# Attention scores head by head on 64x64 quarters of the tensor engine, from plain queries, with shorter first transfers

## The chip, the cores and the metric

The kernel runs on one core of a Trainium2 chip. A core has a tensor engine (PE in the rows; PEld is its weight load), a vector engine (DVE), a scalar engine (ACT), GpSimd (POOL) and a sync engine (SP) that here only issues transfers. The tensor engine has two clock levels, 1.2 and 2.4 GHz; "granted clock 1.00" is the upper one. The metric is the device time of one execution in microseconds, as the median of several runs.

## What is computed

Three stages follow each other: banded attention, a mixture of eight experts with the two best per token, and a dense block. The change is in the first only. Cut to that stage, and to the shape of the others:

```python
batch, n_heads, seq, head_dim = (4, 8, 576, 64)      # q, k, v: float32

def _attn_ref(q, k, v):
    window = 64
    scores = np.matmul(q, k.transpose(0, 1, 3, 2)) / np.sqrt(D)
    rel = pos[:, None] - pos[None, :]
    scores = np.where((rel >= 0) & (rel < window), scores, -1000000000.0)
    attn = np.exp(scores - np.max(scores, axis=-1, keepdims=True))
    attn = attn / (np.sum(attn, axis=-1, keepdims=True) + 1e-09)
    return np.matmul(attn, v)
...
x = attn_out.transpose(0, 2, 1, 3).reshape(B * S, H * D)      # 2304 x 512
x = _moe_ref(x=x, ...)     # router, top 2 of 8 experts, relu(x @ w1) @ w2
return _moe2_ref(x=x, ...) # g(x @ w_in) @ w_out
```

## The kernel before

**Tiling.** The queries of a sequence are cut into 9 blocks of 64 (i), for 4 batch entries (b): 36 steps, s = 4 i + b. A query sees at most the 64 keys of its own block and the 64 before. A step handles all 8 heads, as 4 pairs j of two heads (hi = 0 and 1); head 0 of a pair lies in partitions 0 to 63 and head 1 in 64 to 127, both in what goes in (partition = head dimension) and in the scores (partition = query).

**A step on PE.** First one bf16 matmul writes the mask (identity times mask, 512 columns) into one of three PSUM banks. Then `scores` (L936) adds, for each pair j, one matmul: the weights are a 128x128 block of `q_bd`, block-diagonal with the two heads' queries and zeros elsewhere, and the moving operand is the 128 keys (previous and own block) of both heads from `k_ring`. DVE takes the maximum (L699) and the bias (L704), ACT the exponentials (L552). PE transposes the probabilities (L947), DVE copies them back (L710), `values` (L959) makes eight matmuls with 64-column weights, whose outputs go to partitions 0 to 63 and 64 to 127 of one bank in turn, DVE divides by the sum (L723, `x_blk`), PE transposes x (L969), and every second step it makes the router's logits (L978). The order on PE is written out by hand: scores of step s, transposed probabilities of s-2, values of s-3, transposed x of s-4, logits after even steps. Every float32 matmul against data appears as two records in the trace, transposes as one.

**The first row of steps.** Steps 0 to 3 have no previous block. The kernel still multiplies 128 keys, with the second 64 (block 1, loaded for it at once) masked away; `first_k` therefore loads the keys of blocks 0 and 1, `first_v` the first 128 rows of v, both from ACT's queue. SP loads q, one transfer for each head of a pair, into the diagonal blocks of `q_bd` in runs of 64 numbers, which leaves the zeros that DVE wrote once (L684, L685) in place. Steps 0 and 1 wait for slices of their own, steps 2 and 3 share the third (`row0_loaded`). Each later row waits for `q_loaded` and `k_loaded`. In step b = 1 of each row SP waits until a row of scores is done, and loads q two rows and k three rows ahead. `keep_busy` is a string of matmuls of ones into an unused bank; 12 of them run before step 0.

**Weights beside attention.** POOL fetches the first expert's weights in 1 MB chunks into `stage`, the first two after the third and the sixth group of scores. In 16 pieces ACT casts them (`cast_piece`, L544, in steps 4, 6, ...), and DVE computes the low parts (`low_piece`, L691, in steps 5, 7, ... 35). After the last pieces POOL fetches chunks of the second expert; it converts those itself after the routing (L384). After attention come a routing stage on DVE, and then the experts, in which PE is busy nearly throughout.

Of the kernel before, what the change touches and what calls it, by code (L numbers as in the profile page):

```python
# [27 lines left out]
P = 128  # L28
# [17 lines left out]
def build(nc, qT, kT, vW, noise, w_gate, w_noise, w1, w2, w_in, w_out, out):  # L46
    BLOCKS, _, B, JQ = qT.shape
    Q = 64
    J = JQ // Q
# [31 lines left out]
    with ExitStack() as ctx:  # L81
# [36 lines left out]
        with ExitStack() as s1:  # L118
            sb = sb_in(s1)
            q_bd = sb("q_bd", [P, 2, B, J, 2, Q])  # L120
# [91 lines left out]
        k_loaded = [sem(f"k_loaded{c}") for c in range(4)]  # L212
        v_loaded = [sem(f"v_loaded{b}") for b in range(B)]
# [37 lines left out]
        def _(sp):  # L251
            def load_q(r):
                for hi in range(2):
                    rows = slice(64 * hi, 64 * hi + 64)
                    sp.dma_start(q_bd[rows, r % 2, :, :, hi].rearrange("p b j q -> p (b j) q"),
                                 qT[r, rows].rearrange("p b (j q) -> p (b j) q", j=J)).then_inc(q_loaded[r % 2], 16)
# [29 lines left out]
            for at in (slice(0, 1), slice(1, 2), slice(2, 4)):  # L286
                for hi in range(2):
                    rows = slice(64 * hi, 64 * hi + 64)
                    sp.dma_start(q_bd[rows, 0, at, :, hi].rearrange("p b j q -> p (b j) q"),
                                 qT[0, rows, at].rearrange("p b (j q) -> p (b j) q", j=J)  # L290
                                 ).then_inc(row0_loaded[at.start], 16)
            load_q(1)
            load_k(2)
# [56 lines left out]
        def _(pool):  # L350
# [104 lines left out]
            fetch_first(0, [(scored, 3), (scored, 6)])  # L455
# [82 lines left out]
        def _(act):  # L538
# [7 lines left out]
            def step(s):  # L546
# [16 lines left out]
                if s >= 4 and s % 2 == 0 and s < 4 + 8 * PIECES:  # L563
                    cast_piece((s - 4) // 2)
# [3 lines left out]
            def first_k(at):  # L568
                act.dma_start(k_ring[:, 0:3:2, at], kT[0:2, :, at].rearrange("i p b c -> p i b c")
                              ).then_inc(row0_loaded[at.start], 16)  # L570

            def first_v(b):
                act.dma_start(v_ring[:, b], vW[b, 0:P]).then_inc(v_loaded[b], 16)
# [107 lines left out]
        def _(dve):  # L681

            for c in range(2):
                nc.vector.memset(q_bd[64:128, c, :, :, 0], 0.0).then_inc(zeroed, 1)  # L684
                nc.vector.memset(q_bd[0:64, c, :, :, 1], 0.0).then_inc(zeroed, 1)  # L685

# [9 lines left out]
            def step(s):  # L696
# [30 lines left out]
                if s >= 5 and s % 2 and s < 5 + 8 * PIECES:  # L727
                    low_piece((s - 5) // 2)
# [176 lines left out]
        def _(pe):  # L905
# [7 lines left out]
            keep_busy(banks[7], 12)  # L913
# [263 lines left out]
```

## Time and profile before

| | us |
|---|---|
| median of 3 runs | 1104.11 (1103.42 to 1107.55) |
| profiled execution | 1104.26 |
| its span in the trace | 1102.7 |
| PE busy | 1084.7 (98%) |
| DVE, ACT, POOL busy | 350.1, 345.3, 355.2 |
| first scores, step 4, last logits of attention | from 8.06, 19.58, 121.00 |

The profiled execution is the one whose rows are shown; the time outside its span is 1.6 us. Times in the rows are microseconds from the start of the span. Matmuls are pipelined, so a record's duration includes latency that overlaps its neighbours, and the distance from one group's start to the next is the better measure of what a group costs.

### The profile page before, as it was taken

Reading aid. Unit: us, or ns where it says so; the run is one execution under the profiler, and the core shown is the slowest. Engines: PE = TensorE matmul, PEld = TensorE weight load, DVE = VectorE, ACT = ScalarE, POOL = GpSimd, SP = SyncE. Lnnn points to the kernel's source line nnn. Section 1 sums busy time; section 2 is a strip of 40 time slices with the busy share of each in tenths; the row PEclk is TensorE's granted clock in tenths of the full one; section 3 lists DMA queues with packets and bytes.
Section 4 is the critical chain, followed back from the end, with each engine's and each line's share of the span. In section 5 each row is a group of like instructions: output and inputs, shape, how many; then the busy total and the mean of one; then the engine's idle time right before and its main releaser. Section 6 shows DMA issues by size and latency. Waiting matters only on the chain.

```text
span 1102.7 us, 19553 instructions
## 1 busy us (share of the span) xinstructions
PE 1084.7 (98%) x6669; PEld 934.2 (85%) x6670; DVE 350.1 (32%) x685; ACT 345.3 (31%) x794; POOL 355.2 (32%) x230
## 2 busy tenths in 40 slices
PE   8999899999999999999999999999999999999998
PEld 6999568888888888888888887989989999899897
DVE  5888731122112211221122112424224132241321
ACT  4766212222222222222222221524325244252341
POOL 3000068559644628081725405921010110101000
PEclk8999989999999999999999999999999999999999
DMA  9886445995532514243333402220110201101000
GB/s 234 229 222 167 139 141 192 349 318 191 178 127 76 171 38 152 76 133 114 114 114 98 149 20 88 95 58 16 43 48 9 57 18 39 52 5 57 10 10 20
DMA packets 67844, 120.41 MB, mean 109 GB/s; under 512 B 25632, under 2 KB 30880, under 8 KB 67296
## 3 DMA queue, kind: packets, MB, share of 16 engines
q0 software_dynamic: 16688, 62.66, 17.4%
q1 hardware_dynamic: 37920, 33.67, 10.7%
q10 hardware_dynamic: 13200, 23.60, 6.6%
q8 instruction: 23, 0.38, 0.1%
q14 instruction: 13, 0.11, 0.0%
HBM read 87.14 MB, written 32.77 MB: 109 GB/s over the span
## 4 chain that ended last, share of the span: by engine, by line
PE 91%; POOL 4%; issue 3%; DMA 1%; DVE 0%; SPq 0%; ACT 0%; ACTq 0%; POOLq 0%; DVEq 0%
PE bank L1067 7%; PE bank L1065 7%; PE bank L1066 7%; PE bank L1050 7%; PE bank L1052 7%; PE bank L1051 7%; PE bank L1128 6%; PE bank L1130 6%; PE bank L1129 6%; PE bank L1115 6%; PE bank L1114 6%; PE bank L1113 6%; PE bank L1073 3%; PE bank L936 3%; PE bank L959 2%
## 5 line engine op out<-in xcount | busy, mean ns | idle before, releaser
L386 POOL TENSOR_TENSOR Wl<-stage,Wh 128x2048 fp32r<-128x2048 f32 x36 | 165.8, 4606 | 3.0
L1113 PE MATMUL bank<-zT_h,Wh 128*128 128x256 f32 x576 | 163.0, 283 | 1.0 <-DVE zT_l L873 1.0
L1115 PE MATMUL bank<-zT_h,Wl 128*128 128x256 f32 x576 | 163.0, 283 | 0.0
L1114 PE MATMUL bank<-zT_l,Wh 128*128 128x256 f32 x576 | 163.0, 283 | 0.0
L839 DVE COPY y_out<-bank 128x512 f32<-128x512 f32 x43 | 29.7, 692 | 359.7 <-PE bank L1067 342.4
L1050 PE MATMUL bank<-Wh,xT_h 128*128 x344 | 138.4, 402 | 1.1 <-POOL Wl L386 1.1
L1052 PE MATMUL bank<-Wh,xT_l 128*128 x344 | 134.6, 391 | 0.0
L1065 PE MATMUL bank<-Wh,hT_h 128*128 x344 | 133.9, 389 | 0.4 <-DVE hT_l L843 0.4
L1067 PE MATMUL bank<-Wh,hT_l 128*128 x344 | 134.2, 390 | 0.0
L1051 PE MATMUL bank<-Wl,xT_h 128*128 x344 | 133.8, 389 | 0.0
L1066 PE MATMUL bank<-Wl,hT_h 128*128 x344 | 133.8, 389 | 0.0
L620 ACT ACTIVATE hT_h<-bank 128x512 fp32r<-128x512 f32 x86 | 46.9, 596 | 260.9 <-PE bank L1073 153.4
L887 DVE SCALAR_TENSOR_TENSOR bank<-bank,square 128x512 f32<-128x512 f32 x72 | 50.4, 700 | 219.7 <-ACT square L659 219.7
L384 POOL CAST Wh<-stage 128x2048 fp32r<-128x2048 f32 x36 | 68.4, 1900 | 154.9 <-PE bank L1067 154.7
L502 POOL DMA_INDIRECT y_a<-y_sorted,pair_slot x18 | 17.2, 957 | 303.1 <-PE bank L1100 254.2
L1128 PE MATMUL bank<-Wh,gT_h 128*128 128x512 f32 x288 | 113.0, 393 | 0.2 <-POOL Wl L386 0.2
L1129 PE MATMUL bank<-Wl,gT_h 128*128 128x512 f32 x288 | 112.2, 390 | 0.0
L1130 PE MATMUL bank<-Wh,gT_l 128*128 128x512 f32 x288 | 112.2, 389 | 0.0
L1113 PEld LDWEIGHTS bank<-zT_h,Wh 128*128 128x128 f32 x576 | 110.5, 192 | 1.8 <-issue 1.5
L1114 PEld LDWEIGHTS bank<-zT_l,Wh 128*128 128x128 f32 x576 | 110.6, 192 | 0.3
L1115 PEld LDWEIGHTS bank<-zT_h,Wl 128*128 128x128 f32 x576 | 110.6, 192 | 0.0
L613 ACT ACTIVATE hid<-bank 128x512 f32<-128x512 f32 x86 | 51.4, 599 | 141.2 <-PE bank L1052 141.2
(154 smaller groups left out, 1674.0 us busy)
## 6 DMA issues: line engine op xcount, KB each, us to landing
stage<-w POOLq DMA_DIRECT2D x32, 1024.0 KB
y_sorted<-y_out ACTq DMA_DIRECT2D x43, 256.0 KB
x_in<-x_sorted ACTq DMA_DIRECT2D x39, 256.0 KB
x_sorted<-gath_b SPq DMA_DIRECT2D x20, 256.0 KB
x_sorted<-gath_a SPq DMA_DIRECT2D x19, 256.0 KB
x_rows<-x_blk SPq DMA_DIRECT2D x36, 128.0 KB, 3.0
out<-o_out SPq DMA_DIRECT2D x36, 128.0 KB, 2.2
q_bd<-qT SPq DMA_DIRECT2D x16, 256.0 KB, 4.3
```

Of the source, the lines that this page charges most:

```text
L1050: nc.tensor.matmul(H_ps[a][:], xT_h[:, u, k], high, start=(k == 0), stop=False)
L1051: nc.tensor.matmul(H_ps[a][:], xT_h[:, u, k], low, start=False, stop=False)
L1052: mm = nc.tensor.matmul(H_ps[a][:], xT_l[:, u, k], high, start=False, stop=(k == KD - 1))
L1065: nc.tensor.matmul(Y_ps[:], hT_h[:, k], high, start=(k == 0), stop=False)
L1066: nc.tensor.matmul(Y_ps[:], hT_h[:, k], low, start=False, stop=False)
L1067: mm = nc.tensor.matmul(Y_ps[:], hT_l[:, k], high, start=False, stop=(k == KF - 1))
L1113: nc.tensor.matmul(here, high, zT_h[:, k], start=(k == 0), stop=False)
L1114: nc.tensor.matmul(here, high, zT_l[:, k], start=False, stop=False)
L1115: mm = nc.tensor.matmul(here, low, zT_h[:, k], start=False, stop=(k == KD - 1))
L1128: nc.tensor.matmul(O_ps[u][:], gT_h[:, k, rows], Wh[:, 1, cols], start=(k == 0), stop=False)
L1129: nc.tensor.matmul(O_ps[u][:], gT_h[:, k, rows], Wl[:, 1, cols], start=False, stop=False)
L1130: mm = nc.tensor.matmul(O_ps[u][:], gT_l[:, k, rows], Wh[:, 1, cols], start=False, stop=(k == FC - 1))
```

## The change

The block-diagonal `q_bd` becomes `q_ring`, half as large, loaded by one transfer per slice with 256 to 1024 numbers in a row per partition. `scores` makes two matmuls for each pair of heads, each with a head's 64 partitions of q as 64x64 weights and the same 64 partitions of keys, into the 64 output partitions of that head. In steps 0 to 3 it multiplies 64 keys, and `values` contracts over 64 rows. The first k and v transfers shrink accordingly; k(1), q(1) and the second halves of v for the first row come from SP behind them. The zeroing memsets go. The warm-up matmuls are 9 instead of 12, and two more stand behind each of the first three groups of scores. POOL fetches its first two chunks after score groups 4 and 7, and the pieces of weights are cast and split two steps later.

```diff
-            q_bd = sb("q_bd", [P, 2, B, J, 2, Q])
+            q_ring = sb("q_ring", [P, 2, B, JQ])
...
             def load_q(r):
-                for hi in range(2):
-                    rows = slice(64 * hi, 64 * hi + 64)
-                    sp.dma_start(q_bd[rows, r % 2, :, :, hi].rearrange("p b j q -> p (b j) q"),
-                                 qT[r, rows].rearrange("p b (j q) -> p (b j) q", j=J)).then_inc(q_loaded[r % 2], 16)
+                sp.dma_start(q_ring[:, r % 2], qT[r]).then_inc(q_loaded[r % 2], 16)
...
+                sp.dma_start(q_ring[:, 0, at], qT[0, :, at]).then_inc(row0_loaded[at.start], 16)
+            load_k(1)
             load_q(1)
+            for b in range(B):
+                load_v(b, 1)
             load_k(2)
...
-            fetch_first(0, [(scored, 3), (scored, 6)])
+            fetch_first(0, [(scored, 4), (scored, 7)])
...
-                if s >= 4 and s % 2 == 0 and s < 4 + 8 * PIECES:
-                    cast_piece((s - 4) // 2)
+                if s >= 6 and s % 2 == 0 and s < 6 + 8 * PIECES:
+                    cast_piece((s - 6) // 2)
...
-                act.dma_start(k_ring[:, 0:3:2, at], kT[0:2, :, at].rearrange("i p b c -> p i b c")
-                              ).then_inc(row0_loaded[at.start], 16)
+                act.dma_start(k_ring[:, 0, at], kT[0, :, at]).then_inc(row0_loaded[at.start], 16)
...
-                act.dma_start(v_ring[:, b], vW[b, 0:P]).then_inc(v_loaded[b], 16)
+                act.dma_start(v_ring[0:Q, b], vW[b, 0:Q]).then_inc(v0_loaded[b], 16)
...
-            for c in range(2):
-                nc.vector.memset(q_bd[64:128, c, :, :, 0], 0.0).then_inc(zeroed, 1)
-                nc.vector.memset(q_bd[0:64, c, :, :, 1], 0.0).then_inc(zeroed, 1)
...
-                if s >= 5 and s % 2 and s < 5 + 8 * PIECES:
-                    low_piece((s - 5) // 2)
+                if s >= 7 and s % 2 and s < 7 + 8 * PIECES:
+                    low_piece((s - 7) // 2)
...
-            keep_busy(banks[7], 12)
+            keep_busy(banks[7], 9)
...
                 for j in range(J):
-                    mm = nc.tensor.matmul(
-                        S_ps[s % CH][:, P * j:P * j + P], q_bd[:, i % 2, b, j].rearrange("p a q -> p (a q)"),
-                        k_ring[:, even:odd + 1:odd - even, b, Q * j:Q * j + Q], start=False, stop=True,
-                        skip_group_check=True)
+                    for hi in range(2):
+                        rows, head = slice(Q * hi, Q * hi + Q), slice(Q * j, Q * j + Q)
+                        keys = k_ring[rows, 0, b, head] if i == 0 else k_ring[rows, even:odd + 1:odd - even, b, head]
+                        mm = nc.tensor.matmul(S_ps[s % CH][rows, P * j:P * j + (Q if i == 0 else P)],
+                                              q_ring[rows, i % 2, b, head], keys, start=False, stop=True,
+                                              skip_group_check=True)
...
+                rows = slice(0, Q if i == 0 else P)
...
-                        mm = nc.tensor.matmul(X_ps[s % 2][Q * hi:Q * hi + Q, Q * j:Q * j + Q], probsT[:, head],
-                                              v_ring[:, b, head], start=True, stop=True)
+                        mm = nc.tensor.matmul(X_ps[s % 2][Q * hi:Q * hi + Q, Q * j:Q * j + Q], probsT[rows, head],
+                                              v_ring[rows, b, head], start=True, stop=True)
...
                 if s < G:
                     scores(s)
+                if s < 3:
+                    keep_busy(banks[7], 2)
```

**Where instructions stand, before and after.** The first place is PE's queue at the start, up to the scores of step 3. Before:

```order
L909 MATMUL bank<-ones_b 128x512 x12
L932 MATMUL bank<-mask_first,ident_b 128x512
L936 MATMUL bank<-k_ring,q_bd 128x128 x4
L932 MATMUL bank<-mask_first,ident_b 128x512
L936 MATMUL bank<-k_ring,q_bd 128x128 x4
L932 MATMUL bank<-mask_first,ident_b 128x512
L936 MATMUL bank<-k_ring,q_bd 128x128 x4
L947 MATMUL bank<-ident,probs 128x128 x4
```

PE's queue at the same place after the change:

```order
L901 MATMUL bank<-ones_b 128x512 x9
L921 MATMUL bank<-mask_first,ident_b 128x512
L928 MATMUL bank<-k_ring,q_ring 64x64 x8
L901 MATMUL bank<-ones_b 128x512 x2
L921 MATMUL bank<-mask_first,ident_b 128x512
L928 MATMUL bank<-k_ring,q_ring 64x64 x8
L901 MATMUL bank<-ones_b 128x512 x2
L921 MATMUL bank<-mask_first,ident_b 128x512
L928 MATMUL bank<-k_ring,q_ring 64x64 x8
L901 MATMUL bank<-ones_b 128x512 x2
L938 MATMUL bank<-ident,probs 128x128 x4
```

Three of the ones matmuls left the front, six stand between the score groups, and each score group is eight matmuls of a quarter. The second place is one steady step on PE (scores, transposed probabilities, values, transposed x, logits). Before:

```order
L932 MATMUL bank<-mask_odd,ident_b 128x512
L936 MATMUL bank<-k_ring,q_bd 128x128 x4
L947 MATMUL bank<-ident,probs 128x128 x4
L959 MATMUL bank<-v_ring,probsT 64x64 x8
L969 MATMUL bank<-ident,x_blk 128x2x64 x2
L978 MATMUL bank<-w_gn,xT_blk 128x16 x4
```

The same steady step on PE after the change:

```order
L921 MATMUL bank<-mask_odd,ident_b 128x512
L928 MATMUL bank<-k_ring,q_ring 64x128 x8
L938 MATMUL bank<-ident,probs 128x128 x4
L954 MATMUL bank<-v_ring,probsT 64x64 x8
L964 MATMUL bank<-ident,x_blk 128x2x64 x2
L973 MATMUL bank<-w_gn,xT_blk 128x16 x4
```

The order within a step is the same; only the score group has other shapes, still with 128 keys each. The third place is DVE's queue at the end of attention, steps 37 and 38 of its loop. Before:

```order
L710 COPY probsT<-bank 128x512
L715 TENSOR_SCALAR rowsum_g<-rowsum 128x4
L718 RECIPROCAL rowinv<-rowsum_g 128x4
L723 TENSOR_TENSOR x_blk<-bank,rowinv 128x256
L715 TENSOR_SCALAR rowsum_g<-rowsum 128x4
L718 RECIPROCAL rowinv<-rowsum_g 128x4
L723 TENSOR_TENSOR x_blk<-bank,rowinv 128x256
```

DVE's queue at the same place after the change:

```order
L702 COPY probsT<-bank 128x512
L707 TENSOR_SCALAR rowsum_g<-rowsum 128x4
L710 RECIPROCAL rowinv<-rowsum_g 128x4
L715 TENSOR_TENSOR x_blk<-bank,rowinv 128x256
L683 TENSOR_TENSOR Wl<-stage,Wh 128x512
L707 TENSOR_SCALAR rowsum_g<-rowsum 128x4
L710 RECIPROCAL rowinv<-rowsum_g 128x4
L715 TENSOR_TENSOR x_blk<-bank,rowinv 128x256
```

The last low piece of weights (`Wl`) now stands between the last two blocks of x.

## Rows read from the trace of the kernel before

**Rows 1.** The page's first part: busy us, share of the span, instructions.

```profile
PE 1084.7 (98%) x6669; PEld 934.2 (85%) x6670; DVE 350.1 (32%) x685; ACT 345.3 (31%) x794; POOL 355.2 (32%) x230
```

**Rows 2.** Busy time by stretch, two steady steps, and the first of them alone.

```profile
core 0: us, PE busy (x) PEld busy (x) DVE busy (x) ACT busy (x) POOL busy (x), PEclk, DMA share, GB/s
59.82:62.35 2.53, 2.53 (x34) 2.26 (x31) 2.46 (x6) 1.70 (x9) 0.00 (x0) 1.00 0.82 279
...
59.82:65.68 5.86, 5.86 (x72) 5.32 (x70) 4.88 (x14) 4.01 (x20) 0.00 (x0) 1.00 0.51 160
```

**Rows 3.** Waits from 30 to 100 us: who waited for whom, total, times, longest.

```profile
PEld bank L959 <- issue: 4.0, 24, 0.2
```

**Rows 4.** PE in order of time, a steady step: start, duration of the group, instruction.

```profile
59.82 0.38 PE L932 MATMUL bank<-mask_even,ident_b 128*128 128x512 bf16 x1
60.04 1.05 PE L936 MATMUL bank<-k_ring,q_bd 128*128 128x128 f32 x8
60.93 0.60 PE L947 MATMUL bank<-ident,probs 128*128 128x128 f32 x4
61.46 0.69 PE L959 MATMUL bank<-v_ring,probsT 128*64 128x64 f32 x16
62.07 0.44 PE L969 MATMUL bank<-ident,x_blk 128*128 128x128 f32 x2
62.35 0.96 PE L978 MATMUL bank<-w_gn,xT_blk 128*128 128x16 f32 x8
```

**Rows 5.** PE in order of time, from the start to step 4.

```profile
1.23 4.17 PE L909 MATMUL bank<-ones_b 128*128 128x512 bf16 x12 [1.23 <-POOL ones_b L410]
8.06 0.59 PE L932 MATMUL bank<-mask_first,ident_b 128*128 128x512 bf16 x1 [2.66 <-POOL upper L434]
...
10.96 0.61 PE L932 MATMUL bank<-mask_first,ident_b 128*128 128x512 bf16 x1 [0.61 <-DMA q_bd<-qT]
...
13.94 0.61 PE L932 MATMUL bank<-mask_first,ident_b 128*128 128x512 bf16 x1 [0.67 <-DMA q_bd<-qT]
...
19.58 0.39 PE L932 MATMUL bank<-mask_odd,ident_b 128*128 128x512 bf16 x1
```

**Rows 6.** POOL, DVE and ACT in order of time, around step 0.

```profile
2.73 0.72 POOL L418 TENSOR_SCALAR_AFFINE_SELECT mask_first<-mask_first 64x128 bf16<-64x128 bf16 x2
...
10.39 0.69 DVE L699 TENSOR_REDUCE negmax<-bank 128x4 f32<-128x512 f32 x1 [4.68 <-PE bank L936]
...
12.61 0.21 ACT L552 ACTIVATION_READ_ACCUMULATOR probs<-bank,bias 128x1 f32 x1
```

**Rows 7.** DMA from 0 to 8 us: packets; issues, KB each, median us to landing.

```profile
DMA packets 1774, 1.44 MB, mean 180 GB/s; under 512 B 916, under 2 KB 1428, under 8 KB 1774
...
q_bd<-qT SPq DMA_DIRECT2D x4, 64.0 KB, 6.1
```

**Rows 8.** DVE and PE in order of time, the end of attention.

```profile
119.07 0.42 DVE L723 TENSOR_TENSOR x_blk<-bank,rowinv 128x256 f32<-128x256 f32 x1
...
119.89 0.42 PE L969 MATMUL bank<-ident,x_blk 128*128 128x128 f32 x2
```

**Rows 9.** Value and score records by line, 60 to 66 us: ns min/median/max.

```profile
L959 PE MATMUL bank<-v_ring,probsT x32: 222/222/270, 61.5 to 65.3; 128*64 128x64 f32 x32
...
L936 PE MATMUL bank<-k_ring,q_bd x17: 270/275/275, 60.0 to 65.9; 128*128 128x128 f32 x17
```

**Rows 10.** Busy time by stretch near the start; columns as in rows 2.

```profile
7.00:9.00 2.00, 0.94 (x4) 0.88 (x5) 0.00 (x0) 0.00 (x0) 1.59 (x7) 0.63 1.07 334
8.00:11.50 3.50, 2.83 (x11) 2.39 (x12) 0.86 (x2) 0.18 (x1) 2.20 (x9) 0.50 1.11 301
12.00:15.00 3.00, 2.33 (x11) 1.95 (x11) 0.86 (x2) 1.58 (x11) 0.00 (x0) 0.50 1.41 196
7.00:8.00 1.00, 0.00 (x0) 0.00 (x0) 0.00 (x0) 0.00 (x0) 0.80 (x4) 0.76 1.03 359
17.00:18.00 1.00, 1.00 (x7) 0.91 (x6) 0.82 (x2) 0.78 (x5) 0.86 (x1) 0.62 1.04 397
```

**Rows 11.** POOL in order of time: the second expert's first chunk.

```profile
154.94 1.90 POOL L384 CAST Wh<-stage 128x2048 fp32r<-128x2048 f32 x1
```

More of the change, by code:

```diff
@@ L212, in build @@
         k_loaded = [sem(f"k_loaded{c}") for c in range(4)]
+        v0_loaded = [sem(f"v0_loaded{b}") for b in range(B)]
         v_loaded = [sem(f"v_loaded{b}") for b in range(B)]
@@ L286, in _ @@
             for at in (slice(0, 1), slice(1, 2), slice(2, 4)):
[L287 to L290, printed above, removed]
-                                 ).then_inc(row0_loaded[at.start], 16)
+                sp.dma_start(q_ring[:, 0, at], qT[0, :, at]).then_inc(row0_loaded[at.start], 16)
+            load_k(1)
             load_q(1)
+            for b in range(B):
+                load_v(b, 1)
             load_k(2)
@@ L919, in scores @@
                 if i == 0:
-                    pe.wait_ge(row0_loaded[min(b, 2)], 48)
+                    pe.wait_ge(row0_loaded[min(b, 2)], 32)
                 elif b == 0:
-                    pe.wait_ge(q_loaded[i % 2], 32 * ((i + 1) // 2))
-                    if i >= 2:
-                        pe.wait_ge(k_loaded[i % 4], 16 * ((i + 2) // 4 if i % 4 >= 2 else i // 4))
-                if s in (0, B):
-                    pe.wait_ge(zeroed, 2 * i + 2)
+                    pe.wait_ge(q_loaded[i % 2], 16 * ((i + 1) // 2))
+                    pe.wait_ge(k_loaded[i % 4], 16 * (i // 4 + (1 if i % 4 else 0)))
                 if s in (B, 2 * B):
@@ L952, in values @@
                 pe.wait_ge(pT_copied, s + 1)
-                pe.wait_ge(v_loaded[b], 16 * max(i, 1))
+                if i == 0:
+                    pe.wait_ge(v0_loaded[b], 16)
+                else:
+                    pe.wait_ge(v_loaded[b], 16 * i)
+                rows = slice(0, Q if i == 0 else P)
                 if s >= 2:
@@ L998, in _ @@
             pe.wait_ge(const_ready, ALL_CONSTANTS)
-            pe.wait_ge(zeroed, 5)
+            pe.wait_ge(zeroed, 1)
             keep_busy(banks[4], 28)
```

1 line of the change is left out of this document (removed).

## The prediction

> **What bounds the kernel now.** I read the page first: the tensor engine (PE) is busy 98% of a span of 1102.7 us, so time is lost or won where PE's work gets longer or shorter, or where PE stands still [rows 1]. The change touches only the attention stage, the first 120 us. I read that stage in three pieces.
>
> The steady part is steps 4 to 35. In two consecutive steps, from 59.82 to 65.68 us, PE is busy 5.86 of 5.86 us at a granted clock of 1.00, DVE 4.88 and ACT 4.01 [rows 2]. The only waits on PE's side between 30 and 100 us are 0.2 us at a time of its weight loads in front of the value products, and they wait for no other engine [rows 3]. So PE's queue is the bound here: a step without logits takes 2.53 us, one with them 0.80 more (5.86 for the two), and every 0.1 us on PE in each of 32 steps is 3.2 us of the total.
>
> The start is bound by loads. PE idles 2.66 us before its first mask matmul at 8.06; the next two start at 10.96 and 13.94, and for these the trace names the q transfer as releaser [rows 5]. Step 4, the first on the steady rhythm, starts at 19.58. At the first mask the trace names a POOL instruction, but the constants that it needs (seven, ending with the two mask selects at 2.73) were ready by 3.5 us [rows 6]; what came last must be the transfers. The first four q transfers, of only 64 KB each, land a median of 6.1 us after issue [rows 7].
>
> The end of attention, to about 122 us, is a chain of latencies in which DVE and PE alternate [rows 8].
>
> **Part 1: scores on quarters, steps 4 to 35.** Before, four matmuls of 128x128 weights make 8 records; they hold PE from 60.04 to 60.93, 0.89 us, or 0.111 us a record [rows 4]. After, eight matmuls, each 64 rows by 64 columns of weights, still stream 128 keys, so they make 16 records as long as the old ones. The new q columns have no zeros, but the streaming is per key and not per useful product: if two quarters never ran at once the group would double. No row of this trace shows two quarters on different rows. The nearest are the value products: 128-row by 64-column halves, left and right in turn. A single record there takes 222 ns against 275 for a score record [rows 9], so 53 ns less for half of the streamed columns: 64 keys' worth of streaming is 53 ns, and 128 are 107. Sixteen value records alone would need 16 x 0.053 = 0.85 us; the group goes from 61.46 to the next group's start at 62.07, 0.61 us [rows 4]. So halves that write different partitions of one bank do overlap in pairs. I take it that the diagonal quarters do too: 16 x 0.107 / 2 = 0.85 us of streaming, what it was before.
>
> What comes on top is read from the same value group. The transposes before it are 4 records of 0.107 (0.43 us) and start at 60.93, so they should end at 61.36, and values start at 61.46: 0.10 us. From 61.36 to 62.07 is 0.71 us for 0.43 us of paired streaming (half of 0.85): 0.28 us over. The transposes of x behind it take 0.28 (62.07 to 62.35) where two records are 0.21, another 0.06 [rows 4]. Between groups of full-width weights there is next to nothing: mask to scores 0.22 for 512 bf16 columns (0.213), scores to transposes 0.89 for 0.85. So entering and leaving the split array costs 0.28 to 0.34 us per group. The scores group sits between a full-width mask and full-width transposes, so it pays the same: 0.85 + 0.28 to 0.34 = 1.13 to 1.19 us against 0.89, so +0.24 to +0.30, and I add about 0.01 because the half-filled first and last slot is longer for a longer record. I take **+0.28 us a step, x 32 = +9.0 us**. Bounds: no switching cost and full overlap, +0 to +0.03 a step (0 to +1 us); no overlap, 16 x 0.111 = 1.78 plus the 0.2 of the two switches, 1.98, so +1.09 a step (+35 us).
>
> Cover: DVE has 4.88 us of work in 5.86, ACT 4.01 [rows 2]. A longer PE step only widens that margin.
>
> **Part 2: the start.** Four edits act here. The first transfers carry half the keys and half the values of the first row of steps: q 0.5 MB, k 0.5, v 0.5 instead of 0.5, 1.0 and 1.0. The q transfer is one per slice instead of two, with runs of 1 KB or 4 KB per partition instead of 256 B. From 12 to 15 us, with the 256-byte runs of q(1) in flight, the DMA share was 1.41 at only 196 GB/s; from 7 to 9 us it was 1.07 at 334 [rows 10]. The four memsets of q's zeros leave DVE, which then waited 4.68 us for the first scores [rows 6]: worth nothing. The score products of steps 0 to 3 stream 64 keys: 8 x 2 records at 53 ns.
>
> Step 2 needs all of q(0) and k(0), 1.0 MB, and what the two queues interleave with it, some 0.4 MB of v and k(1). By rows 7, 1.44 MB had moved by 8.0 us, so step 2 can start near **7.5 us** instead of 13.94, steps 0 and 1 near 4.7 and 6 (twelve warm-up matmuls end at 5.4 in rows 5, the last ones at 0.22 each as the mask in rows 4, so nine end at about 4.7). Step 4 needs k(1) and q(1) too: 2.5 MB in all, which had moved at about 11.5 us before (1.44 MB to 8.0, then 3.5 us at 301 GB/s, 1.0 MB more [rows 10]), with under 1 us to land: **12.2 us** instead of 19.58. The engines' latency allows that: from the end of step 0's scores, where the first reduction starts, to its last exponential are 2.4 us (10.39 to 12.82) [rows 6], so the exponentials of step 0 end at about 8.2, transposes 0 and scores 3 follow from 8.6 to 9.8, and scores 4, after transposes 1 and values 0, could start at 11.2. The six extra warm-up matmuls (0.43 us a pair) fall in these waits. The gain is 19.58 - 12.2 = **-7.4 us**. Upper end -8.4, if only the latencies bind. Lower end -4: the granted clock was below full in the slice from 7 to 8 us, after PE had been idle from 5.4, and back in the slice from 17 to 18 [rows 5, 10]. A cold step costs some 2.5 us more; if the clock falls again in the short gaps between the first steps, one or two of the steps from 4 on run at half clock.
>
> SP's queue: k(1), q(1), four v transfers, k(2), k(3) and the small loads stand ahead of the first per-step wait. They are 14 issues where there were 13, of fewer descriptors; the first that has to wait is needed at step 8 only, near 23 us. POOL's first weight chunk waits for four score groups instead of three, but that falls at about 10 instead of behind the third group's end near 16, so it meets k(1), q(1) and v. ACT needs it in step 6 only, near 20 us. Nothing.
>
> **Part 3: the pieces of weights, two steps later.** The last DVE piece (0.68 us) moves from step 35 to step 37, between the x block of step 34 and that of step 35. There x_blk of step 35 runs from 119.07 to 119.49, and PE, busy with logits, takes it up at 119.89 [rows 8]. The piece puts x_blk's end at about 120.2, PE follows at 120.3: **+0.4 us** (0 to +0.7). POOL's next chunk is fetched some 3 us later and first converted at 154.9 [rows 11], so it is not late. From there on the program is the same, and the whole shift arrives at the end.
>
> **Sum.** -7.4 + 9.0 + 0.4 = +2.0 us on the profiled execution's 1104.26 (span 1102.7 and 1.6 around it), which is 0.15 above the median of 1104.11. **Forecast 1106.3.**
>
> **Rivals.** (a) *The quarters take turns.* The two quarters of a pair write one bank from different rows of the array; the value halves, the only rows that show an overlap, share both bank and rows [rows 4]. If quarters don't overlap, part 1's bound holds: +35 us for 32 steps, with -7.4 and +0.4: **1132**. Page "TensorEngine Tiling (Array Packing)" of the Trainium skill, Gotcha 1, is a rule for it: different row tiles cannot access the same PSUM bank simultaneously; no row here shows two row tiles. It decides once more than an eighth of the pairs fail to overlap (0.81 us x 32 = 26 us for all of them; 3.5 would carry the sum past +5.5). Against it: the two quarters write different partitions, as the halves of rows 4 do. 0.15.
> (b) *Switching is free here.* If the 0.28 to 0.34 us of the value group belongs to its three semaphore waits and not to the split, the scores, which wait for nothing after the mask, pay +1 us in all: -7.4 + 1 + 0.4 = **1098.3**. Against it: the 0.06 behind the group is no wait, and groups headed by a mask or transposes wait as well at almost no cost. 0.20.
> (c) *The start gives little*, as k(1) and q(1) land with the chunk in front of them or the clock falls: -4 + 9 + 0.4 and a little, **1110 to 1111**. 0.12.
> The forecast's own case has 0.53, from 1104 (+0.24 a step, -8.4) to 1110.5 (+0.34, a start of -5).
>
> **How the numbers follow.** A measurement of this kernel tells about 0.5% (5.5 us) from no change: 1098.6 to 1109.6. Rival (b) straddles the lower edge: 0.12 of it is faster, and 0.06 I take from the forecast's case for a gain that I don't see, with fewer q packets: faster 0.18. Slower is (a), most of (c), and the forecast's upper tail: 0.15 + 0.08 + 0.07 = 0.30. Same 0.52. The range of 8 in 10 leaves out (a) and the outer ends: 1098 to 1114. The likeliest case alone is 1104 to 1110.5.
>
> **What would show it.** In the new trace: score records in pairs, 16 in about 1.0 us, and transposes of the probabilities starting about 1.17 us after the first quarter; if they start 1.9 or more after, (a). A plain step of 2.81, one with logits of 3.62; if 2.55, (b). The mask of step 4 at 12.2; at 15 or later, (c). x_blk of step 35 behind a weight piece. I would be wrong beyond all this if PE waited for DVE in the steady part, or if the stages behind attention did not start with the same delay.

## The result

| | before | after |
|---|---|---|
| median of 5 runs, us | 1104.11 (1103.42 to 1108.55) | 1113.78 (1111.72 to 1114.69) |
| profiled execution, its span, us | 1104.26, 1102.7 | 1111.87, 1110.3 |
| mask of step 4 | 19.58 | 15.33 |
| steady: a plain step, and two steps with logits once | 2.53, 5.86 | 2.80, 6.42 |
| transposed x of step 35 | 119.89 | 124.52 |
| first routing matmul on PE | 128.79 | 135.94 |

The ratio over all the runs is 1.0068 (95% interval 1.005 to 1.0086), so the kernel is slower by some 7.5 us. The two medians lie further apart, 9.7 us, because the five runs of before fall in two clumps, three from 1103.42 to 1104.11 and two at 1107.55 and 1108.55 (the last section comes to that). The forecast was no change, at 1106.3. The median lies just inside the range of 1098 to 1114, and beyond the likeliest case's own 1110.5.

The page's first part (engine: busy us, share of the span, instructions), against [rows 1], has 8.7 us more of PE work, about what 32 steps got longer:

```profile
PE 1093.4 (98%) x6960; PEld 926.6 (83%) x6961; DVE 347.6 (31%) x681; ACT 345.0 (31%) x794; POOL 355.2 (32%) x230
```

Busy time by stretch, a plain step and then two steps, against [rows 2]:

```profile
core 0: us, PE busy (x) PEld busy (x) DVE busy (x) ACT busy (x) POOL busy (x), PEclk, DMA share, GB/s
59.49:62.29 2.80, 2.80 (x41) 2.09 (x39) 2.69 (x8) 1.57 (x9) 0.00 (x0) 1.00 0.48 162
59.49:65.91 6.42, 6.42 (x88) 5.06 (x86) 4.93 (x14) 4.01 (x20) 0.00 (x0) 1.00 0.42 121
```

PE in order of time in the same step (start, duration of the group, instruction), against [rows 4]:

```profile
59.49 0.38 PE L921 MATMUL bank<-mask_even,ident_b 128*128 128x512 bf16 x1
59.80 1.09 PE L928 MATMUL bank<-k_ring,q_ring 64*64 64x128 f32 x16
60.82 0.66 PE L938 MATMUL bank<-ident,probs 128*128 128x128 f32 x4
61.41 0.69 PE L954 MATMUL bank<-v_ring,probsT 128*64 128x64 f32 x16
62.02 0.44 PE L964 MATMUL bank<-ident,x_blk 128*128 128x128 f32 x2
62.30 0.96 PE L973 MATMUL bank<-w_gn,xT_blk 128*128 128x16 f32 x8
```

Start to start, against before: mask to scores 0.31 (was 0.22), scores to transposes 1.02 (0.89), transposes to values 0.59 (0.53). These three make the 0.28. PE is never idle, at a granted clock of 1.00.

PE at the start, against [rows 5]:

```profile
5.04 0.63 PE L921 MATMUL bank<-mask_first,ident_b 128*128 128x512 bf16 x1
...
7.05 0.38 PE L921 MATMUL bank<-mask_first,ident_b 128*128 128x512 bf16 x1
...
11.31 0.39 PE L921 MATMUL bank<-mask_first,ident_b 128*128 128x512 bf16 x1 [2.73 <-DMA k_ring<-kT]
...
15.33 0.39 PE L921 MATMUL bank<-mask_odd,ident_b 128*128 128x512 bf16 x1
```

Steps 0 and 1 start at 5.04 and 7.05, where 4.7 and 6 were forecast, and step 2 at 11.31 and not at 7.5. The DMA issues from 0 to 8 us (count, KB each, median us to landing), against [rows 7], name what it waited for:

```profile
q_ring<-qT SPq DMA_DIRECT2D x1, 256.0 KB, 4.8
k_ring<-kT ACTq DMA_DIRECT2D x1, 256.0 KB, 8.8
```

The third slice of q landed 4.8 us after its issue, the slice of k of the same size 8.8 us.

The end of attention, DVE and then PE in order of time, against [rows 8]:

```profile
122.69 0.42 DVE L715 TENSOR_TENSOR x_blk<-bank,rowinv 128x256 f32<-128x256 f32 x1
123.03 0.68 DVE L683 TENSOR_TENSOR Wl<-stage,Wh 128x512 fp32r<-128x512 f32 x1
...
124.04 0.42 DVE L715 TENSOR_TENSOR x_blk<-bank,rowinv 128x256 f32<-128x256 f32 x1
```

```profile
123.45 0.96 PE L973 MATMUL bank<-w_gn,xT_blk 128*128 128x16 f32 x8
124.52 0.44 PE L964 MATMUL bank<-ident,x_blk 128*128 128x128 f32 x2
125.65 1.64 PE L973 MATMUL bank<-w_gn,xT_blk 128*128 128x16 f32 x8 [0.69 <-ACT xT_blk L558]
127.12 8.98 PE L901 MATMUL bank<-ones_b 128*128 128x512 bf16 x28
135.94 0.23 PE L999 MATMUL bank<-picked,upper 128*128 128x152 bf16 x1
```

Behind x come the last logits, 28 filler matmuls of ones, and the routing's first matmul, which needs `picked` from DVE (133.66 to 133.97). In the trace of before the same rows, not shown so far, read:

```profile
119.08 0.96 PE L978 MATMUL bank<-w_gn,xT_blk 128*128 128x16 f32 x8
119.89 0.42 PE L969 MATMUL bank<-ident,x_blk 128*128 128x128 f32 x2
121.00 1.06 PE L978 MATMUL bank<-w_gn,xT_blk 128*128 128x16 f32 x8 [0.69 <-ACT xT_blk L561]
121.91 6.20 PE L909 MATMUL bank<-ones_b 128*128 128x512 bf16 x28
128.79 0.24 PE L1002 MATMUL bank<-picked,upper 128*128 128x152 bf16 x1 [0.68 <-DVE picked L770]
```

From x of step 35 to the routing it is 8.90 us there and 11.42 here. The stretches of after say why: the granted clock was at the lower level from about 126 us to 132.8, in before's trace at 1.00 until the routing.

```profile
126.00:128.00 2.00, 2.00 (x10) 1.45 (x10) 0.54 (x2) 0.00 (x0) 0.00 (x0) 0.50 0.71 283
```

The same 28 fillers took 8.98 us instead of 6.20, and now PE, not DVE, came last: DVE's `picked` ends 9.45 us behind x instead of 8.85, which is 0.6 of the 2.5 us, and PE's overrun is the rest. So the trace's account, after against before: -4.25 at step 4; +8.7 over the 31 steps to the mask of step 35 (114.50 against 110.06), which makes +4.44 there; +4.36 at the values of step 35 (122.42 against 118.06); +4.63 with the piece of weights; +7.15 at the routing; +7.6 at the end of the span.

### The profile page after: what moved, and what is told of

It reads as the page before. It is cut to its first block, busy times and chain, and to the rows that moved or that the text cites. A ratio compares the mean times of both kernels' runs of the same rounds, so it can differ in the third digit from the quotient of the medians.

```text
span 1110.3 us, 20125 instructions
## 1 busy us (share of the span) xinstructions
PE 1093.4 (98%) x6960; PEld 926.6 (83%) x6961; DVE 347.6 (31%) x681; ACT 345.0 (31%) x794; POOL 355.2 (32%) x230
## 4 chain that ended last, share of the span: by engine, by line
PE 93%; POOL 3%; DVE 1%; issue 1%; DMA 1%; ACT 0%; ACTq 0%; DVEq 0%; POOLq 0%
PE bank L1047 7%; PE bank L1049 7%; PE bank L1062 7%; PE bank L1064 7%; PE bank L1048 7%; PE bank L1063 7%; PE bank L1125 6%; PE bank L1127 6%; PE bank L1126 6%; PE bank L1112 6%; PE bank L1111 6%; PE bank L1110 6%; PE bank L1070 3%; PE bank L928 3%; PE bank L954 2%; PE bank L938 2%
```

## Experiments

The theory behind the first four runs: 0.28 us a step belongs to the score group's quarters alone and is the price of going from full-width weights to split ones and back. Rivals: the longer steps come from the loads or the moved pieces, or from the new record shape whatever its neighbours. Each group of runs had its own runs of before beside it: 19 with a median of 1106.06 for the first four, 25 with 1105.09 for the next four, 24 with 1105.91 for the last three. Ratios are comparable across groups, medians less so. "Better than the changed kernel" below is the difference of the two ratios, in us of 1104; the changed kernel's own interval is 1.005 to 1.0086, so a difference of less than some 3 us is not shown by the times alone.

**Quarters alone.** The kernel before with plain queries and the new score loop; transfers, sizes and everything else as before.

```diff
-            q_bd = sb("q_bd", [P, 2, B, J, 2, Q])
+            q_ring = sb("q_ring", [P, 2, B, JQ])
...
-                    mm = nc.tensor.matmul(
-                        S_ps[s % CH][:, P * j:P * j + P], q_bd[:, i % 2, b, j].rearrange("p a q -> p (a q)"),
...
+                    for hi in range(2):
...
+                        mm = nc.tensor.matmul(S_ps[s % CH][rows, P * j:P * j + P], q_ring[rows, i % 2, b, head],
...
```

> The kernel before with one part of the change alone: the scores as eight quarter products from plain q (q still loaded in runs of 256 bytes, all first transfers, warm-ups and weight pieces as before). Theory: the +0.28 us a step on PE is the score group alone (0.89 us to about 1.2), so steps 4 to 35 give +9.0 us, step 4 still starts near 19.6, and the time is 1104.1 + 9 = 1113, plus up to 2.5 if the clock falls behind attention as it did in the changed kernel. Rival: part of the +0.28 comes from elsewhere (the weight pieces two steps later, other DMA traffic); then the plain step stays under 2.75 us and the time under 1110.

Measured: 1114.41 us (1113.35 to 1115.74), ratio 1.0087 (1.0064 to 1.0111), which is +9.6 us. PE in its steady step:

```profile
59.69 0.38 PE L927 MATMUL bank<-mask_even,ident_b 128*128 128x512 bf16 x1
59.99 1.09 PE L933 MATMUL bank<-k_ring,q_ring 64*64 64x128 f32 x16
...
62.49 0.38 PE L927 MATMUL bank<-mask_even,ident_b 128*128 128x512 bf16 x1
```

2.80 from mask to mask, as in after. The quarters alone make the loss. Step 4 starts at 18.32 in this trace, 1.26 earlier than in before's, though nothing in its loads was changed: one profiled start is not yet its program's start.

**Start alone.** The changed kernel with the block-diagonal queries and full-width weights back.

```diff
-            q_ring = sb("q_ring", [P, 2, B, JQ])
+            q_bd = sb("q_bd", [P, 2, B, J, 2, Q])
...
+                    mm = nc.tensor.matmul(S_ps[s % CH][:, P * j:P * j + (Q if i == 0 else P)],
+                                          q_bd[:, i % 2, b, j].rearrange("p a q -> p (a q)"), keys, start=False,
...
```

> The changed kernel with the other part alone: block-diagonal q and four 128x128 score products a step as before (64 keys in steps 0 to 3), with the shortened first transfers, the fillers and the later weight pieces. Theory: steady steps are back at 2.53 and 3.33 us; step 4 starts 4 us earlier than before if what delayed it is the order and share of the transfers, so 1104.1 - 4 + 0.3 = 1100. Rival: the plain q transfers were what brought the 4 us (the q slices of 256-byte runs land late again), then step 4 starts at 17 or later and the time is 1102 to 1104.

Measured: 1104.80 us (1101.64 to 1106.42, 10 runs), ratio 0.9993 (0.9978 to 1.0009): the whole start is worth 0.8 us, between 2.4 of gain and 1 of loss. The time expected above is 4.8 lower, and the times include the later pieces (some +0.3). A plain step is back at 2.52 (60.26 to 62.78). At the start no load holds PE up for long, and step 4 comes before the rival's 17, but PE is slow:

```profile
5.96 1.80 PE L940 MATMUL bank<-k_ring,q_bd 128*128 128x64 f32 x8
...
14.70 1.00 PE L940 MATMUL bank<-k_ring,q_bd 128*128 128x64 f32 x8
...
16.69 0.39 PE L934 MATMUL bank<-mask_odd,ident_b 128*128 128x512 bf16 x1
```

The same eight records take 1.80 us in step 0, 1.81 in steps 1 and 2, and 1.00 in step 3. The masks of steps 1 and 2 take 0.63 us, as at the lower clock in before's trace (0.61 at a granted clock of 0.50), and this trace's first clock record, at the upper level, begins at 13.9 us, where after's begins at 6.5. So the lower clock lasted longer here than in after's trace, with the same nine warm-up matmuls; why is open. Step 4 starts at 16.69, 2.9 earlier than before and not 7.4. Quarters and start together, +9.6 - 0.8 = +8.8, agree with the +7.5 of the whole change within the intervals.

**By rows.** The changed kernel with the four upper quarters first and the four lower ones then.

```diff
-                for j in range(J):
-                    for hi in range(2):
+                for hi in range(2):
+                    for j in range(J):
```

> The changed kernel, with the eight quarter products of a step in another order: the four of the upper rows first, then the four of the lower rows. Theory: two quarters overlap only because neighbours in the queue lie on different quarters, starts being in order; four in a row on one quarter run one after the other, 16 x 0.107 = 1.7 us, +0.8 us a step, 1113.8 + 27 = 1140. Rival: the queue finds the other quarter's work by itself, then the time stays within 3 us of 1113.8.

Measured: 1125.78 us (two runs, 1123.78 and 1127.78), ratio 1.019 (1.0155 to 1.0226). Its score group:

```profile
61.31 1.58 PE L928 MATMUL bank<-k_ring,q_ring 64*64 64x128 f32 x16
62.82 0.66 PE L938 MATMUL bank<-ident,probs 128*128 128x128 f32 x4
```

1.51 us to the transposes against 1.02: neither theory's number, but in between. The starts of the single records show why. In after's trace they are two files of eight, both from 59.80 or 59.81 to 60.61 or 60.62. Here the upper quarters' file runs from 61.31 to 62.13 and the lower ones' from 61.81 to 62.62: the second starts 0.49 us late, which is the whole difference, and while three records of the first have yet to start. So the two files overlap in part even when they stand one behind the other in the queue, and wholly only when they alternate. Without any overlap the streaming alone would be 16 x 0.107 = 1.7 us, an estimate from [rows 9].

**Values first.** The changed kernel with the values of step s-3 ahead of the transposes of step s-2, so that the two split groups (scores and values) are neighbours.

```diff
-                if 2 <= s < G + 2:
-                    transposed_probs(s - 2)
                 if 3 <= s < G + 3:
                     values(s - 3)
+                if 2 <= s < G + 2:
+                    transposed_probs(s - 2)
```

> The changed kernel with the value products placed in front of the transposes of probabilities in each step on PE, so that the two split groups (64x64 scores, 128x64 values) stand next to each other: three changes of the array's division a step instead of four. Theory: the price is the change of division, so one of four falls away, -0.1 us a step or more, -3 to -5 us: 1109 to 1111. Rival 1: a change between two kinds of split costs the same as two changes from and to the full array, or the price lies in the split groups' own records: no difference. Rival 2: the later transposes make DVE's copy late, and PE waits: slower.

Measured: 1105.41 us (1102.81 to 1108.77, 10 runs), ratio 1.0003 (0.9988 to 1.0017), 7.2 us better than the changed kernel, where 3 to 5 were expected. PE in its steady step:

```profile
62.17 0.38 PE L921 MATMUL bank<-mask_even,ident_b 128*128 128x512 bf16 x1
62.48 1.09 PE L928 MATMUL bank<-k_ring,q_ring 64*64 64x128 f32 x16
63.50 0.69 PE L954 MATMUL bank<-v_ring,probsT 128*64 128x64 f32 x16
64.12 0.66 PE L938 MATMUL bank<-ident,probs 128*128 128x128 f32 x4
...
64.83 0.38 PE L921 MATMUL bank<-mask_odd,ident_b 128*128 128x512 bf16 x1
```

2.66 a step instead of 2.80, 4.5 us over 32 steps; from the mask of step 4 (17.10) to the transposed x of step 35 (120.99) it is 103.89 us against 109.19, so another 0.8 comes at the end, where the chain of latencies is shorter. The remaining 1.9 of the 7.2 is within the intervals.

**The same swap in the kernel before** (one run) is the control. There the scores are full width, and the swap joins nothing.

> The kernel before, with the value products in front of the transposes of probabilities on PE. Here the scores are full-width, so the array is divided and joined once a step in either order. Theory (the price is per change of division): a plain step stays within 0.05 us of 2.53. Rival (the order itself, or the waits at the head of the value products, made the 0.14 us a step that the same swap gave the changed kernel): 2.40 or less.

Measured: 1107.64 us in one run. A step with logits goes from 60.71 to 64.05, 3.34 us, and [rows 2] give 5.86 - 2.53 = 3.33: no change. From scores to values it is 0.99 us, where [rows 4] have 0.89 from scores to transposes: the 0.10 us ahead of the value group moved with it. So, as far as one trace of each kernel shows, the swap's 0.14 us is the price of one change from split weights to full ones and back, which is what the theory says. This trace shows another thing too: it has the fall of the clock behind attention, without any quarter.

```profile
121.49 1.89 PE L978 MATMUL bank<-w_gn,xT_blk 128*128 128x16 f32 x8 [0.69 <-ACT xT_blk L561]
123.22 8.49 PE L909 MATMUL bank<-ones_b 128*128 128x512 bf16 x28
```

**What held the third slice of k.** Two theories: SP's later transfers (k(1), q(1), v) compete with it for the DMA engines; or it stands in ACT's own queue behind the first slice of v. First run: SP holds its later loads until the slice has landed. Second: k's slice goes ahead of v in ACT's queue.

```diff
+            sp.wait_ge(row0_loaded[2], 32)
             load_k(1)
             load_q(1)
```

> The changed kernel, with SP's second group of transfers (k(1), q(1), the second halves of v, k(2), k(3) and the small loads) issued only when the third slices of q(0) and k(0) have landed. In the changed kernel step 2 starts at 11.31 us and waits for the third slice of k, which lands 8.8 us after its issue. Theory: that slice shares the DMA engines with what SP issues behind q(0); held back, it lands by about 8 and step 2 starts at 7.5 to 8.5, step 4 at 12 to 13.5, so about 2 to 3 us less than the changed kernel in the trace. Rival: the slice is held up in ACT's own queue behind the first slice of v, then step 2 still starts after 10, and step 4 gets later as k(1) and q(1) come late.

```diff
-                first_v(0)
                 first_k(slice(2, 4))
+                first_v(0)
```

> The changed kernel, with ACT issuing the third slice of k in front of the first slice of v instead of behind it; SP's transfers as in the changed kernel. Theory (SP's transfers take the share): step 2 still starts at 10 or later. Rival (ACT's own queue): step 2 starts by 9.

Measured: held loads 1112.29 us (1109.35 to 1115.69), ratio 1.0057 (1.0034 to 1.0079); k first 1109.06 us (1108.04 to 1113.10), ratio 1.0044 (1.0024 to 1.0064). Issues and PE's start, first with held loads, then with k first:

```profile
k_ring<-kT ACTq DMA_DIRECT2D x1, 256.0 KB, 6.8
...
9.31 0.39 PE L922 MATMUL bank<-mask_first,ident_b 128*128 128x512 bf16 x1 [0.88 <-DMA k_ring<-kT]
...
14.69 0.39 PE L922 MATMUL bank<-mask_odd,ident_b 128*128 128x512 bf16 x1 [1.29 <-DMA q_ring<-qT]
```

```profile
k_ring<-kT ACTq DMA_DIRECT2D x1, 256.0 KB, 6.6
...
8.55 0.39 PE L921 MATMUL bank<-mask_first,ident_b 128*128 128x512 bf16 x1 [0.37 <-DMA k_ring<-kT]
...
13.33 0.39 PE L921 MATMUL bank<-mask_odd,ident_b 128*128 128x512 bf16 x1 [0.69 <-DMA q_ring<-qT]
```

Both bring step 2 forward, by 2.0 and 2.8 us; in the four traces whose program is after's up to step 2 it starts at 10.45 (bridges, below), 11.31, 11.65 (fewer fillers, below) and 11.86 (values first), so both are beyond that spread. Both theories hold a part, and the own queue holds more. Neither cure is free: held loads make step 4 wait 1.29 us for q(1), and k first 0.69 us, as q(1) now lands 10.4 us after its issue instead of 8.8. With k first, step 4 starts at 13.33, 2.0 earlier than in after's trace, 6.25 earlier than before, and 1.1 later than the forecast's 12.2. Against the changed kernel the times are 1.2 us (held loads) and 2.7 us (k first) better, neither clear of the intervals.

**A bridge over the end of attention.** The changed kernel with two ones matmuls behind steps 36, 38 and 40, where PE waits.

```diff
+                if s in (G, G + 2, G + 4):
+                    keep_busy(banks[0], 2)
```

> The changed kernel, with two matmuls of ones (0.43 us) in front of each of the three places where PE waits at the end of attention (steps 36, 38 and 40 of its loop). In the changed kernel the granted clock falls to 0.5 at about 126 us, the last logits take 1.64 us instead of 1.06, and the 28 warm-up matmuls behind them take 8.98 us instead of 6.20 and end 2 us after DVE has what they stand in front of. Theory: PE's idle time of about 2 us from 118 to 126 lets the clock fall; filled, it stays at 1.00 until the routing's own gap, the last logits are back at 1.06 us and the time falls by 2 to 2.5 us, to 1111.5. Rival: the fall has to do with what the array did before (quarters), not with the gaps; then it still falls and the time stays at 1113.8 or above.

Measured: 1110.68 us (1108.40 to 1112.36), ratio 1.0046 (1.0030 to 1.0062). The clock fell all the same, later and for half as long:

```profile
124.78 1.06 PE L973 MATMUL bank<-w_gn,xT_blk 128*128 128x16 f32 x8 [0.26 <-ACT xT_blk L558]
125.69 7.89 PE L901 MATMUL bank<-ones_b 128*128 128x512 bf16 x28
```

The logits are back at 1.06, the fillers at 7.89 between 6.20 and 8.98. In the trace the stretch from x to the routing is 9.77 us instead of 11.42, 1.65 better, and another 0.86 is an earlier step 4 (14.47), which the bridges can't have made. The times are 2.4 us better, as expected, but that is within the intervals, and the mechanism held only half.

**Fewer fillers.** The changed kernel with 18 fillers instead of 28, so that PE's queue ends before DVE's pick even at the lower clock.

```diff
-            keep_busy(banks[4], 28)
+            keep_busy(banks[4], 18)
```

> The changed kernel with 18 instead of 28 warm-up matmuls in front of the first matmul of the routing, nothing else. In the changed kernel's trace they end at 135.9 while DVE's result stood at 134.0. Theory: this overrun is what the fallen clock costs, the first routing matmul follows DVE within 0.3 us, -1.5 to -2 us against 1113.8. Rival: the clock falls again behind them, no gain.

Measured: 1110.62 us (1110.23 to 1111.26), ratio 1.0055 (1.0037 to 1.0073), 1.4 us less than the changed kernel, within the intervals; PE does wait for DVE again (1.14 us, for `picked`), and the stretch from x to the routing is back at 8.91 us, though the clock fell here too (18 fillers took 5.73 us). More telling is its start. Up to the fillers its program is that of after, instruction for instruction:

```profile
6.91 0.61 PE L901 MATMUL bank<-ones_b 128*128 128x512 bf16 x2
11.65 0.61 PE L921 MATMUL bank<-mask_first,ident_b 128*128 128x512 bf16 x1 [4.13 <-DMA k_ring<-kT]
12.19 1.12 PE L928 MATMUL bank<-k_ring,q_ring 64*64 64x64 f32 x16
...
18.29 0.39 PE L921 MATMUL bank<-mask_odd,ident_b 128*128 128x512 bf16 x1
```

Step 2 comes at 11.65, almost as in after (11.31), but at the lower clock (score group 1.12 us for 0.68), and step 4 at 18.29 for 15.33. The same program has a start worth -4.25 in one execution, -1.3 in another, and -5.1 in the bridge's.

**Both halves where they pay.** Steps 0 to 3 as quarters from plain queries (in the k slot that is still free), from step 4 on block-diagonal queries at full width, k ahead of v, values first, and two of the bridges. In a second kernel 20 fillers besides.

```diff
+                for j in range(J if i >= 1 else 0):
...
+                    mm = nc.tensor.matmul(S_ps[s % CH][:, P * j:P * j + P],
+                                          q_bd[:, i % 2, b, j].rearrange("p a q -> p (a q)"),
...
+                for j in range(J if i < 1 else 0):
+                    for hi in range(2):
...
-                                              q_ring[rows, i % 2, b, head], keys, start=False, stop=True,
+                                              k_ring[rows, 3, b, head], keys, start=False, stop=True,
...
```

> What the runs so far say is good, put together: steps 0 to 3 as in the changed kernel (plain q, here parked in a free slot of the k ring, quarters, 64 keys, short first transfers, the third k slice in front of the first v slice), from step 4 on the block-diagonal q and full-width scores of the kernel before, value products in front of the transposes of probabilities, two matmuls of ones in front of steps 38 and 40. Theory: step 4 starts near 13.5 to 14.5 (19.58 before), a plain step is 2.53 us, the end of attention is 0.8 shorter by the swap; -5.5 - 0.8 and up to 2.5 for the clock: 1097 to 1100 where the kernel before has 1104 to 1105. Rival: q(1), in runs of 256 bytes, lands late, or the clock falls near 12 us as in half of the runs; then step 4 starts at 16 or later and the time is 1101 to 1103.

> The same, with 20 instead of 28 warm-up matmuls in front of the first matmul of the routing. When the clock is at half there, 28 of them take 7.8 to 9 us and end up to 2 us after DVE has what they stand in front of; 20 take 8.5 at most. Theory: 1 to 2 us less than with 28 when the clock falls behind attention, nothing when it doesn't. Rival: the fewer warm-ups leave PE idle for longer and the clock falls once more behind them, then the routing gets longer and the time is the same or more.

Measured: 1102.29 us (1099.29 to 1104.33, 12 runs), ratio 0.9968 (0.9953 to 0.9984); with 20 fillers 1102.72 us (1099.21 to 1105.15, 12 runs), ratio 0.9976 (0.9961 to 0.9991). Both are faster than both kernels, by 3.5 and 2.7 us against before, and the times are those of the rival, 1101 to 1103. The first one's PE:

```profile
7.51 0.39 PE L929 MATMUL bank<-mask_first,ident_b 128*128 128x512 bf16 x1
...
15.23 0.61 PE L929 MATMUL bank<-mask_odd,ident_b 128*128 128x512 bf16 x1 [3.56 <-DMA q_bd<-qT]
15.63 1.92 PE L934 MATMUL bank<-k_ring,q_bd 128*128 128x128 f32 x8
```

Step 2 stands at 7.51, the number of the forecast. Now q(1), in runs of 64 numbers again, is late (256 KB per head, landed after a median of 11.0 us), PE idles 3.56 us, and the clock is at the lower level from 14.6 to 21.4 us. So of the 4.35 us that step 4 is earlier than in before's trace, 1.64 are left at the transposed x of step 35 (118.25 against 119.89). A plain step is 2.53. With 20 fillers the clock did not fall behind attention in the profiled execution (4.48 us of fillers at a granted clock of 1.00, then 2.40 us of waiting for DVE), so that trace doesn't test them, and the times show no difference.

## Why the forecast missed

The range held, by 0.2 us at the median. That is luck more than foresight: in the trace the start gave 3.15 us less than the sum has, and the end of attention took 2.5 more.

**Score quarters, +9.0: right in size.** +0.28 a step; plain step 2.80 (2.81), with logits 3.62 (3.62). Its place is another than sketched: the forecast had all of it between the first quarter and the transposes (1.17 us), the trace has 0.09 ahead of the group, 0.13 in it (1.02) and 0.06 behind it. The reading of the value group as the price of a split was right in mechanism, which the swap shows by halving it. Rival (a) is refuted: 16 records run in 1.09 us and start in pairs, 0.01 us apart, where one behind the other they would need 1.7. Gotcha 1 of "TensorEngine Tiling (Array Packing)" in the Trainium skill says that different row tiles cannot access one PSUM bank at the same time, which would rule the overlap out; the measured diagonal quarters write different partitions of one bank and overlap, so here the measurement decides against it. Rival (b) is refuted by the same 0.28.

**Start, -7.4: the failed step.** In the trace it is -4.25. The term took bytes in flight as a common pool, and the bytes did move no later than counted (1.69 MB by 8.0 us, 2.88 by 12.0). But step 2's k slice was not among the early ones: it stood behind a slice of v on ACT's queue, and moving it gave step 2 at 8.55 and step 4 at 13.33. Two of the three missing microseconds are shown by that run. From step 2 to step 4 it took 4.0 us; the forecast's latencies gave 3.7 (7.5 to 11.2) and its loads 4.7.

The late slice may well cost a second time, through the clock. Seven traces have the changed kernel's start, two of them with one of the cures above. In four of them PE idled 0.37, 0.88, 1.90 and 2.73 us before step 2 (k first, held loads, bridges, after); the granted clock stayed at 1.00, and step 4 started between 13.33 and 15.33. In the other three it idled 2.84, 3.73 and 4.13 us (by rows, values first, fewer fillers); the clock was at the lower level from 12.0, 12.2 and 11.0 us on, and step 4 started at 17.44, 17.10 and 18.29. This is an order among seven traces and no shown threshold: quarters alone, with other transfers, idled 1.52 and then 2.09 us, and its clock fell at 12.3. The low end of -4 and rival (c) had that clock in them, at a chance of 0.12; it should have been the main case.

What the start is worth in the times stays open. In the traces an earlier step 4 does arrive: from there to the transposed x of step 35 it is 108.9 to 109.2 us in four traces with the changed kernel's steps (after, quarters alone, bridges, fewer fillers), wherever step 4 stands, and 109.7 and 110.0 in the two with moved loads. From the first routing matmul to the end of the span it is 973.1 to 975.1 us in all thirteen. But the profiled start differs from one execution to the next by up to 3.8 us for one program, and the times say only this: start alone, pieces included, -0.8 us, between -2.4 and +1.0, with -2.9 at step 4 in its trace; after against quarters alone, which differ in the start and the pieces, 0.19% or -2.1 us, with some 3 us to either side by an estimate from the two intervals.

**Pieces, +0.4: right in kind.** Without the piece PE would have gone from logits to x in 0.81 us as before; it took 1.07, so +0.26.

**Not in the sum.** "From there on the program is the same, and the whole shift arrives at the end" failed in the trace: +4.6 became +7.15, by the clock's fall behind attention and fillers whose count was cut for the upper clock. The thirteen traces sort this stretch, from the transposed x of step 35 to the routing. It is 8.90 to 8.92 us in before's and in the two with 18 or 20 fillers; 9.75 to 9.77 in five whose clock was low half as long as after's (start alone, by rows, k first, bridges, mixed); and 11.08 to 11.42 in after's, quarters alone, both swaps and held loads. Eleven of the thirteen have a low stretch there. Before's profiled execution is one of the two that have none, so the forecast was laid on the rarer case among these.

That is shown for the traces. For the medians it is not: before's program with the swap has the fall as well, bridges and fewer fillers shorten the stretch but their times are not clear of the changed kernel's, and I can't say how much of the 7.5 us is due to it. The three terms as profiled give -4.25 + 9.0 + 0.3 = +5.0 (the trace has +4.63 at x), just under the interval's lower edge of 5.5. With start alone's time in the place of start and pieces it is 9.0 - 0.8 = +8.2, which is inside; but these times have in them whatever the clock did, so this doesn't show that the fall costs nothing.

**Forecast from one execution.** The sum was laid on 1104.26. Over all 68 runs of before beside the experiments the medians are 1105.1 to 1106.1, so 1 to 2 us of the miss in medians lay in the base.

## What to carry over

Price a split of the array by its borders: lay split groups side by side, and alternate between quarters within one, so that two quarters' streaming always overlaps. At a start bound by loads, follow each transfer in its own queue instead of adding up bytes, and write down what the start is worth if the clock falls, since the execution that was profiled need not be the usual one. A filler that is counted in instructions gets longer when the clock falls (28 of them took 6.20, 7.89 or 8.98 us), so let it end before what it bridges.

## What the runs showed of the hardware

- Diagonal quarters (64 rows by 64 columns) that write different partitions of one bank overlap in pairs, 16 records in 1.09 us; with the four upper ones first it is 1.58, and the lower quarters' first record starts 0.49 us behind the upper ones' first, before the last three of those.
- A change between full-width and split weights cost about 0.28 us a group, in and out; two split groups as neighbours save 0.14. This is float32, one trace for each order.
- The granted clock at the start and behind attention differs between executions. Within the changed kernel's start the three traces with the longest idle time before step 2 are those that fell to the lower level, but that isn't the whole of it: in after's trace PE idled 2.73 us and came back at the upper level, in that of quarters alone 2.09 us and came back at the lower (mask 0.61 us).
- Before's runs go with the mean granted clock of the execution: in the first group of 19, nine have 1102.96 to 1104.21 us at 0.992 to 0.995, ten 1106.06 to 1107.99 at 0.989 to 0.991. A clock lower by 0.004 is 0.004 x 1104 = 4.4 us, and the clumps' medians lie 3.5 apart. In the other groups they run into each other. What sets it stays open.
- Issue to landing at the start hangs on the place in the queue: the same 256 KB slice of k took 8.8 us behind a 128 KB slice of v (7.9 and 9.1 in two more executions), 6.6 ahead of it, and 6.8 behind it with SP quiet.
